# The first layers of two MLPs by Strassen's method with seven products, on tiles of 768 tokens, with streamed weights

## What is computed

```python
def _moe_ref(x, w1, w2, w3, w_out):        # 512 -> 1024 (twice), product, 1024 -> 1024 -> 512
    a = x @ w1
    b = x @ w2
    h = a * b @ w3
    return (h @ w_out).astype(np.float32)

def _moe2_ref(x, w_in, w_out):             # 512 -> 2048 -> 512
    h = x @ w_in
    g = h * (1.0 / (1.0 + np.exp(-h)))
    return (g @ w_out).astype(np.float32)
```

## Time and profile before

| | us |
|---|---|
| Median of 3 runs (lowest, highest) | 880.03 (879.86, 880.94) |
| The profiled execution's own time | 880.67 |
| Its span, first to last instruction | 878.9 |
| TensorE busy in the span | 858.4 |
| Attention phase | 0 to about 173 |
| First MLP, second MLP | 173 to about 474, about 474 to 876 |
| Mean granted clock of TensorE | 0.995 |

### The profile page before, as it was taken

The page is one execution under the profiler, slowest core; times in us unless marked ns, Lnnn a source line. Parts: engine busy times, 40 slices in busy tenths (PEclk is TensorE's granted clock), DMA queues, the critical chain, the costliest instruction groups (busy, mean ns, idle before and its releaser), DMA issues.

```text
span 878.9 us, 15422 instructions
## 1 busy us (share of the span) xinstructions
PE 858.4 (98%) x5872; PEld 792.3 (90%) x5872; DVE 317.5 (36%) x628; ACT 246.1 (28%) x584; POOL 143.8 (16%) x186
## 2 busy tenths in 40 slices
PE   5899999999999999999999999999999999999998
PEld 4678888899999999999999999999999999999997
DVE  4667777755212222121124432322222222322321
ACT  3656556433312222131224322111111111111211
POOL 5776566344000000000024000000000000000000
PEclk9899999999999999999999999999999999999999
DMA  7856665470000000000143000000000001000000
GB/s 192 207 128 160 172 160 141 100 204 0 2 1 0 0 0 0 0 1 1 49 139 100 1 1 37 1 1 36 0 0 36 0 0 37 1 0 33 4 1 37
DMA packets 90310, 43.54 MB, mean 50 GB/s; under 512 B 61856, under 2 KB 82848, under 8 KB 90272
## 3 DMA queue, kind: packets, MB, share of 16 engines
q1 hardware_dynamic: 90272, 43.01, 18.5%
HBM read 38.27 MB, written 4.72 MB: 49 GB/s over the span
## 4 chain that ended last, share of the span: by engine, by line
PE 94%; DVE 2%; POOL 1%; issue 1%; ACT 0%; DMA 0%; DVEq 0%; SPq 0%; POOLq 0%
PE ps L799 80%; PE ps L907 5%; PE ps L889 2%; PE ps L824 2%; PE ps L873 1%; PE ps L834 1%; PE ps L845 1%; PE ps L915 1%; POOL r L360 1%; PE ps L864 1%; PE ps L856 1%; DVE r L663 0%; DVE x L654 0%; DMA qn<-in_q 0%; DVE tot L701 0%
## 5 line engine op out<-in xcount | busy, mean ns | idle before, releaser
L799 PE MATMUL ps<-xs,r 128*128 128x384 f32 x2304 | 425.0, 335 | 0.1
L799 PEld LDWEIGHTS ps<-xs,r 128*128 128x128 f32 x2304 | 405.1, 188 | 8.7 <-issue 0.4
L799 PE MATMUL ps<-r,gh 128*128 128x512 f32 x576 | 194.9, 392 | 0.0
L585 ACT ACTIVATE gf<-ps 128x384 f32<-128x384 f32 x96 | 47.2, 492 | 320.0 <-PE ps L799 320.0
L766 DVE CAST gh<-gf 128x384 fp32r<-128x384 f32 x96 | 35.0, 364 | 281.6 <-ACT gf L585 274.7
L799 PEld LDWEIGHTS ps<-r,gh 128*128 128x128 f32 x576 | 108.1, 188 | 20.3 <-issue 0.2
L799 PE MATMUL ps<-r,gl 128*128 128x512 f32 x288 | 113.7, 395 | 0.0
L799 PE MATMUL ps<-gh,r 128*128 128x384 f32 x384 | 97.3, 334 | 0.0
L732 DVE TENSOR_TENSOR gf<-ps,osb 128x384 f32<-128x384 f32 x48 | 26.7, 557 | 186.7 <-ACT osb L431 186.7
L431 ACT ACTIVATE osb<-ps 128x384 f32<-128x384 f32 (+1 forms) x60 | 30.8, 513 | 194.9 <-PE ps L799 194.9
L799 PEld LDWEIGHTS ps<-gh,r 128*128 128x128 f32 x384 | 69.3, 188 | 0.0
(11 more groups left out here) (71 smaller groups left out, 648.4 us busy)
## 6 DMA issues: line engine op xcount, KB each, us to landing
raw<-in_moe_w_out SPq DMA_DIRECT2D x24, 256.0 KB, 3.0
qn<-in_q SPq DMA_DIRECT2D x32, 144.0 KB, 2.8
kn<-in_k SPq DMA_DIRECT2D x32, 144.0 KB, 3.2
vw<-in_v SPq DMA_DIRECT2D x32, 144.0 KB, 3.0
out<-osb SPq DMA_DIRECT2D x18, 256.0 KB, 2.0
wn<-in_moe_w SPq DMA_DIRECT2D x16, 256.0 KB, 3.2
raw<-in_moe_w SPq DMA_DIRECT2D x16, 256.0 KB, 4.5
raw<-in_moe_w_in SPq DMA_DIRECT2D x16, 256.0 KB, 4.9
```

What stands on the lines that cost most here:

```text
L585: nc.scalar.activation(gf[:, n % 2, :], ps[:, n % 2, 0:T], ACT.Silu).then_inc(g_ready, 1)
L799: e = nc.tensor.matmul(o, weights[a][l], tile[a][r], start=(first and a == 0 and p == 0), stop=(last and a == kk - 1 and p == 2))
```

## The change

T becomes 768, so there are three tiles. The first layers are computed by Strassen's method in Winograd's form. Tokens are cut in halves of 384, inputs in halves of 256 and output features in two blocks of 128; a **set** is such a 2 x 2 block product of seven products instead of eight. Each product is six matmuls of 384 columns. There are 24 sets in the first MLP (even k from w1, odd k from w2; 8 to a tile) and 24 in the second (8 to a tile).

- Weights are no longer kept: rw holds the raw blocks of a set (two buffers), loaded by SyncE, GpSimd makes four sums (`sums`), ScalarE the high parts of all seven factors (`weights_high`, 1792 columns in one operation) and GpSimd the low parts (`weights_low`, 1792 columns). The weights of the output layer are streamed in the same way (`out_weights_high`, `out_weights_low`).
- Tokens: seven factors a tile (xb). VectorE makes four sums (`sum_tokens`, `more_sums`), ScalarE all high parts (`tokens_high`), VectorE the low parts 0, 1, 3, 5 and GpSimd 2, 4, 6 (`tokens_low`), 768 columns each, during the last set of the tile before.
- The seven products use two PSUM banks in turn. ScalarE takes the first product (`take_m1`) and the first quarter (`take_c11`), VectorE adds the others up (`add`). TensorE waits before each product for what frees its bank.
- For the product a*b VectorE has `multiply` and `hidden_low` in odd sets, ScalarE `hidden_high`. In the second MLP it is `silu` and `split_g`.
- `L2_PARTS`, `L2_LAST` and `L4_PARTS` say how many parts of the following layer stand behind each product. A part of `l2` is three matmuls of 512 or of 256 columns, a part of `l4` three of 512.
- In the attention phase GpSimd has `sums(0)` at the head of the last step that computes scores, and the last step is put in another order on TensorE, ScalarE and VectorE. Buffers are laid out anew. The MLPs are written out without loops.

The diff, cut to what matters; 12 columns of indent are taken off:

```diff
-    T = 384
+    T = 768
+    TH = T // 2
+    PRODUCTS = 7
+    A_SLOT = (1, 4, 2, 5, 3, 0, 6)
+    QUARTERS = (0, 3, 2, 1)
+    GROUPS = TILES * MT // 2
+    SETS1 = 2 * GROUPS
+    SETS2 = TILES * FT // 2
+    SETS = SETS1 + SETS2
+    PER = 8
+    STAGES = SETS // PER
+    assert KT == HP == 4 and N % T == 0 and MT == PER and FT // 2 == PER
+    WIDE = 512
+    REST = T - WIDE
...
+        L2_PARTS = (0, 1, 2, 1, 2, 1, 2, 1, 2, 1, 2, 1, 0, 0)
+        L2_LAST = (0, 2, 3, 3, 3, 3, 2)
+        L4_PARTS = (1, 2, 2, 2, 2, 2, 1)
...
+def load_weights(k):
+    w = ((w1, w2)[k % 2] if k < SETS1 else w_in).rearrange("(k p) n -> p k n", p=P)
+    m, far = (k % PER // 2, MT // 2) if k < SETS1 else (k % PER, FT // 2)
+    after(sp, wa_lo, k - 1)
+    for b, n in ((0, m + far), (1, m)):
+        sp.dma_start(rw[:, k % 2, 2 * b:2 * b + 2, :].rearrange("p a (k c) -> p (a k) c", c=P),
+                     w[:, :, n * P:(n + 1) * P]).then_inc(rw_in[k % 2], 16)
...
+def sums(k):
+    blocks = rw[:, k % 2, :, :]
+    pool.wait_ge(rw_in[k % 2], 32 * (k // 2) + 32)
+    nc.gpsimd.tensor_tensor(blocks[:, 4, :], blocks[:, 0, :], blocks[:, 1, :], ALU.add
+                            ).then_inc(s1_ready, 1)
+    nc.gpsimd.tensor_tensor(blocks[:, 6, :], blocks[:, 2, :], blocks[:, 0, :], ALU.subtract
+                            ).then_inc(s3_ready, 1)
+    pool.wait_ge(s1_ready, k + 1)
+    nc.gpsimd.tensor_tensor(blocks[:, 5, :], blocks[:, 4, :], blocks[:, 2, :], ALU.subtract
+                            ).then_inc(s2_ready, 1)
+    pool.wait_ge(s2_ready, k + 1)
+    nc.gpsimd.tensor_tensor(blocks[:, 7, :], blocks[:, 3, :], blocks[:, 5, :], ALU.subtract
+                            ).then_inc(s4_ready, 1)
+def weights_low(k):
+    pool.wait_ge(wa_hi, k + 1)
+    nc.gpsimd.tensor_tensor(wa[:, k % 2, 1, :, :], rw[:, k % 2, 1:8, :],
+                            wa[:, k % 2, 0, :, :].bitcast(F32), ALU.subtract).then_inc(wa_lo, 1)
+def tokens_low(v, n):
+    pool.wait_ge(xb_hi, 7 * v + n + 1)
+    nc.gpsimd.tensor_tensor(xb[:, n, 1, :, :], tokens(v, n), xb[:, n, 0, :, :].bitcast(F32),
+                            ALU.subtract).then_inc(xb_lo[n], 1)
...
+    if not turn:
+        sums(0)
...
+tokens_low(0, 2)
+weights_low(0)
+tokens_low(0, 4)
+tokens_low(0, 6)
+for k in range(SETS):
+    if k + 1 < SETS:
+        sums(k + 1)
+        weights_low(k + 1)
+    if k >= SETS1:
+        out_weights_low(k - SETS1)
+    if k % PER == PER - 1 and k + 1 < SETS:
+        for n in (2, 4, 6):
+            tokens_low((k + 1) // PER, n)
...
+    if last:
         w3_high((MT - 1, 1), pT)
+        tokens_high(0, 1)
+        act.wait_ge(vt_ready, PAIRS)
+        tokens_high(0, 2)
+        act.wait_ge(scored, 2 * PAIRS)
+        act.wait_ge(pooled, 2 * PAIRS)
+        tokens_high(0, 3)
+        act.wait_ge(masked, PAIRS)
+        act.wait_ge(w3_turned, 2 * MT)
+        act.wait_ge(vd_ready, PAIRS)
+        weights_high(0)
...
+for k in range(SETS):
+    v, c, n = k // PER + 1, k % PER, k // 2
+    new = c == PER - 1 and v < STAGES
+    take_m1(k)
+    if k + 1 < SETS:
+        if k == 0:
+            act.wait_ge(w3_mul, MT)
+        weights_high(k + 1)
+    if new:
+        tokens_high(v, 0)
+    to_b = k < SETS1 and k % 2 == 1
+    if to_b:
+        hidden_high(n, 0)
+    else:
+        take_c11(k)
+    if new:
+        act.wait_ge(prod, PRODUCTS * k + 3)
+        tokens_high(v, 1)
+        tokens_high(v, 2)
+    if k >= SETS1:
+        out_weights_high(k - SETS1)
+        silu(k, 1)
+    elif to_b:
+        hidden_high(n, 1)
+    if new:
+        act.wait_ge(prod, PRODUCTS * k + 5)
+        tokens_high(v, 3)
+        tokens_high(v, 4)
+    if k < SETS1 and c == 1 and k > PER:
+        store_x2(k // PER - 1)
+    if k >= SETS1:
+        silu(k, 2)
+    elif to_b:
+        hidden_high(n, 2)
+    if new:
+        act.wait_ge(prod, PRODUCTS * k + 6)
+        tokens_high(v, 5)
+    if k >= SETS1:
+        silu(k, 3)
+    elif to_b:
+        hidden_high(n, 3)
+    if new:
+        act.wait_ge(prod, PRODUCTS * k + 7)
+        tokens_high(v, 6)
+    if k > SETS1 and c == 0:
+        store_out((k - SETS1) // PER - 1)
+    if k == SETS1:
+        store_x2(TILES - 1)
...
-        split_lo(0, 0, 0)
-        for m in range(HEAD // 2, HEAD):
-            r1_low(m)
+        more_sums(0)
+        tokens_low(0, 0)
+        tokens_low(0, 1)
+        tokens_low(0, 3)
         take_down()
...
+def add(k, i, o, term):
+    dve.wait_ge(prod, PRODUCTS * k + i + 1)
+    nc.vector.tensor_tensor(o, half_bank(k, i), term, ALU.add).then_inc(sum_ready, 1)
+def multiply(n, a):
+    q = QUARTERS[a]
+    dve.wait_ge(sum_ready, 5 * (2 * n + 1) + a + 2)
+    nc.vector.tensor_tensor(a4[:, q, :], mu[:, (0, 1, 0, 2)[q], :], a4[:, q, :], ALU.mult
+                            ).then_inc(h_mul, 1)
+def hidden_low(n, a):
+    q = QUARTERS[a]
+    to = slice(q % 2 * TH, (q % 2 + 1) * TH)
+    dve.wait_ge(h_hi, 4 * n + a + 1)
+    nc.vector.tensor_tensor(g[:, 1, n % 2, q // 2, to], a4[:, q, :], g[:, 0, n % 2, q // 2, to].bitcast(F32),
+                            ALU.subtract).then_inc(h_lo, 1)
...
+for k in range(SETS):
+    v, c, n = k // PER + 1, k % PER, k // 2
+    new = c == PER - 1 and v < STAGES
+    to_b = k < SETS1 and k % 2 == 1
+    dve.wait_ge(m1_ready, k + 1)
+    add(k, 1, mid, m1)
+    if to_b:
+        dve.wait_ge(prod, PRODUCTS * k + 3)
+        dve.wait_ge(c11_taken, n + 1)
+        nc.vector.tensor_tensor(a4[:, 0, :], half_bank(k, 2), a4[:, 0, :], ALU.mult
+                                ).then_inc(h_mul, 1)
+        dve.wait_ge(h_mul, 4 * n + 1)
+    add(k, 3, late, m1)
+    if new:
+        tokens_low(v, 0)
+    dve.wait_ge(sum_ready, 5 * k + 2)
+    add(k, 4, late if to_b else a4[:, 3, :], late)
+    if to_b:
+        multiply(n, 1)
+        hidden_low(n, 0)
+    elif k >= SETS1:
+        split_g(k, 0)
+    if new:
+        tokens_low(v, 1)
+    add(k, 5, m1 if to_b else a4[:, 2, :], m1)
+    if to_b:
+        multiply(n, 2)
+        hidden_low(n, 1)
+    elif k >= SETS1:
+        split_g(k, 1)
+    if new:
+        tokens_low(v, 3)
+    dve.wait_ge(sum_ready, 5 * k + 1)
+    add(k, 6, mid if to_b else a4[:, 1, :], mid)
+    if to_b:
+        multiply(n, 3)
+        hidden_low(n, 2)
+        hidden_low(n, 3)
+    elif k >= SETS1:
+        split_g(k, 2)
+        split_g(k, 3)
+    if new:
+        tokens_low(v, 5)
+    if c == 4 and v < STAGES:
+        sum_tokens(v)
+        more_sums(v)
+    if k < SETS1 and c == 1 and k > PER:
+        store_x2(k // PER - 1)
+    if k == SETS1:
+        store_x2(TILES - 1)
+    if k > SETS1 and c == 0:
+        store_out((k - SETS1) // PER - 1)
...
+def product(k, i):
+    v, c = k // PER, k % PER
+    if i == 0:
+        pe.wait_ge(wa_lo, k + 1)
+        after(pe, sum_ready, 5 * (k - 1) + 4)
+    elif i == 1:
+        after(pe, sum_ready, 5 * k)
+    elif i == 2:
+        pe.wait_ge(m1_ready, k + 1)
+    elif i == 4:
+        if k < SETS1 and k % 2 == 1:
+            pe.wait_ge(h_mul, 4 * (k // 2) + 1)
+        else:
+            pe.wait_ge(c11_taken, k - GROUPS + 1 if k >= SETS1 else k // 2 + 1)
+    else:
+        pe.wait_ge(sum_ready, 5 * k + {3: 1, 5: 2, 6: 3}[i])
+    if c == 0:
+        pe.wait_ge(xb_lo[i], v + 1)
+    for a in range(2):
         for p, (l, r) in enumerate(((0, 0), (1, 0), (0, 1))):
-            e = nc.tensor.matmul(o, weights[a][l], tile[a][r], start=(first and a == 0 and p == 0),
-                                 stop=(last and a == kk - 1 and p == 2))
-    return e
-def ab_part(i, n, z, a):
-    u, m = n // MT, n % MT
-    if z == 0 and a == 0:
-        if u == 0:
-            pe.wait_ge(r1_lo, 2 * m + 2)
-        pe.wait_ge(ab_ready, 2 * MT * i + n + 1)
-    e = product(ps[:, 2 * (n % 2) + z, 0:T], [[r1[:, 2 * m + z, l, a * P:(a + 1) * P] for l in range(2)]],
-                [[xs[:, u % 2, r, a, :] for r in range(2)]], a == 0, a == KT - 1,
-                (2 * i + u, a) if m == 0 and z == 0 else None)
-    if z == 1 and a == KT - 1:
-        e.then_inc(ab_done, 1)
+            e = nc.tensor.matmul(ps[:, (k + i) % 2, 0:TH], wa[:, k % 2, l, A_SLOT[i], a * P:(a + 1) * P],
+                                 xb[:, i, r, a, :], start=(i in (0, 1, 4) and a == 0 and p == 0),
+                                 stop=(a == 1 and p == 2), skip_group_check=True)
+    e.then_inc(prod, 1)
...
+        for a in range(4):
+            multiply(a)
+        multiply(0, (MT - 1, 1))
+        multiply(1, (MT - 1, 1))
         turn_local()
-        multiply(0)
-        multiply(1)
         turn_down()
-        multiply(2)
         weighted_local_waits()
-        multiply(3)
+        multiply(2, (MT - 1, 1))
+        multiply(3, (MT - 1, 1))
         weighted_local()
-        for a in range(4):
-            multiply(a, (MT - 1, 1))
         weighted_down()
-        for z in range(2):
-            for a in range(KT):
-                ab_part(0, 0, z, a)
         return
...
+for k in range(SETS):
+    for i in range(PRODUCTS):
```

(12 more changed lines are left out.)

566 lines of the change are left out of this document (265 added, 301 removed).

## The result

| | before | after |
|---|---|---|
| Median, us | 879.94 | 923.38 |
| Lowest to highest, us | 878.31 to 880.94 | 922.19 to 927.55 |
| Profiled execution's own time (span), us | 880.67 (878.9) | 927.55 (925.7) |

Before's median is here that of its runs beside after's. The ratio is 1.0499, 95% interval 1.0464 to 1.0533. The forecast was 892, with a range of 866 to 909: the sign was right, the size wrong. The profiled execution is the slowest of after, 4 us above its median; against before's it is 46.9 us longer, where the sum said 11.7.

A forecast was written before the change was run, and what follows sets the result against it. TensorE, busy 98% of the span, was taken to bound the kernel. -49.9 + 12 + 16 + 6 + 1.6 + 4 + 5 + 17 = +11.7 us on 880.67 gave 892.4, forecast 892, range 866 to 909.

The forecast's parts named there:

- Matmuls times interval, -49.9: First layers of both MLPs: 288 fewer matmuls of 384 columns at 0.1733 us each save 49.9 us.
- rival b: Second layer of the first MLP: narrow 256-column matmuls cost 0.158 us each, adding 12 us, to 904; chance 0.08.
- Holds on VectorE: VectorE operations with two SBUF inputs wait for GpSimd operations to end; adds, which read PSUM, do not.
- ordinary pair: Two sets of the first MLP without a tile change: 1.5 us lost in each of eight, +12 us.
- Changes of the first MLP: Tile changes at sets 7 to 8 and 15 to 16: product 4 starts late, 8 us each, +16 us.
- Start: Attention's end and first sets: first product at 179.2 us, set 1 at 193.9, +17 us (10 to 22).
- Second MLP, ordinary sets: 0: Second MLP: each add is done 1 us or more ahead because 12 output parts lie between products; 0 us.
- +5 for both: Second MLP, sets 31 and 39: tokens_low come between, walked at 0 to 3.5 us; 5 us for both.
- Clock, 0 in the sum: TensorE's clock falling after waits was left out of the sum and kept only as a rival, chance 0.12.
- (a): Queues keep up: VectorE's two-SBUF-input operations wait little for GpSimd, all lower ends hold, 867 us; chance 0.25.
- (c): Waits at tile changes and start lower TensorE's clock three to five times, +6 to +15 us, up to 907; chance 0.12.
- (d): Whole kernel: the sums cancel the saving within 1.8 us; chance 0.05.

The follow-up runs named there:

- a2_spread: The changed kernel with VectorE's four token sums in the second MLP put one each behind sets 2 to 5 of a tile: 909.92 us, ratio 1.0336 to before.
- a1_sums_first: The changed kernel with GpSimd computing the sums for the set after next ahead of the last tokens_low at four tile changes: 908.14 us, ratio 1.0311 to before.
- c1_wait_long: The kernel before with TensorE made to wait six times in the second MLP for a GpSimd addition of 1024 columns: 908.42 us, ratio 1.0302.
- a14_x2: Reordered changed kernel (spread sums, new start, serving new sets first), with next-layer parts dealt later where they wait for x2 copies: 876.55 us, ratio 0.9948 to before.
- a6_all: The changed kernel with four order edits together (GpSimd sums first, token sums spread, start reordered, l2 parts dealt out evenly): 890.34 us, ratio 1.0108 to before.
- a11_adds: The kernel with four order edits, plus VectorE's add of product 6 ahead of hidden_low(1) and tokens_low(3) at every tile change: 908.54 us, ratio 1.0303 to before.

## Why the prediction was wrong in size

- **Matmuls times interval, -49.9**: right. The 256-wide ones cost what their columns say (rival b, 0.158 each, fell): in the timeline of after three of them start at 300.56 and the next work at 300.91, 0.117 each.
- **Holds on VectorE**: right as a mechanism, adds free and operations with two SBUF inputs held. No row of before showed one behind 4 us; L739 took 4.81 us in place of 0.95 behind one of 4.28. That agrees with the Trainium skill (SBUF — State Buffer, "SBUF: two separate sides"), by which the other "fully blocks". The ordinary pair was 30% too dear: at the end of set 3 only the first hidden_low and the first multiply were held, where I had them held behind every sum.
- **Changes of the first MLP**: 13.3 for 16, but not by the one wait that was walked. Of the 6.7 us of a change, 2.5 stand ahead of product 4 behind a4, where I had all of it, 6.0 to 9.6; the rest is VectorE's adds ahead of products 0 and 1. The sign that I had named, gaps of 3 us or more behind a4, didn't come; that the sum of a change came out near is partly luck.
- **Start**: 14.1 for 17. The first product was walked rightly (178.56 against 179.2). That set 1 starts at 194.07, as forecast (193.9), is luck: I had it wait for weights_low(1), which ended at 193.00 with TensorE still at work. What delayed it were the waits of products 3 and 4 of set 0 and 2.3 us of slow clock, which the sum hadn't. Up to there gaps cost 10.8 where I had 13.2, and the end of set 1 cost 3.3 where I had 5.5.
- **"Second MLP, ordinary sets: 0"**: this step failed. The 12 parts of the output layer do cover the adds, but the set in which the token sums stand isn't ordinary: 10.5 us. a2_spread shows it.
- **"+5 for both" changes of the second MLP**: mis-sized, 11.2. The walk stopped at VectorE and left out the late sums (a1_sums_first brings the two to 5.3) and the copies to osb.
- **Clock, 0 in the sum**: this step failed most, 20.0 us. I treated the fall as a rival of 3 to 5 times with a price of 2 to 3 us; it was twelve times at 1.55 to 2.3. Eight of the twelve lie at places that my own sum had as waits: the start, sets 8, 16 and 24, and the copies of x2 in sets 10, 18 and 25. Two more are at sets 29 and 37, two at the changes of the second MLP. With 1.55 on each of the twelve, the sum would have been near 30 instead of 12. The Trainium skill (TensorE: Matmul & The Clock Gate, "Why this matters for your kernels") warns of idle gaps between bursts; I weighed it, and gave it 0.12. The gaps of 2.5 to 2.7 us that brought the clock down in c1_wait_long are shorter than those it warns of, and the measurement decides. c1_wait_long also shows the price.
- **What offset what**: clock +20.0, sets 29 and 37 +10.5, changes of the second MLP +6.2 and smaller gaps +8 over the forecast; ordinary pairs -3.6, start -2.9, changes of the first MLP -2.7 under it. The waits alone, without the clock, sum to 69 us against the 49.9 saved, so the sign doesn't hang on the clock.
- **Rivals**: (a) the queues keep up: fell. That the queues can be made to keep up well enough is shown by a14_x2, with edits of order only. (c) was right as a mechanism, with 20.0 us where it had 6 to 15, and ran on top of the forecast, not in its place. (d), the sums cancelling, fell with the sign. I had put the forecast's losses and the clock's as alternatives, though the one causes the other.

## What to carry to other kernels

A gap ahead of TensorE of 2.5 us or more costs itself and, mostly, 1.6 us of slow clock: put both into the sum for each one, and count the gaps just under 2 us as open (four of 1.7 to 1.9 us in after were followed by a fall, two of 1.8 us weren't). When work leaves the bounding engine and goes to the others, walk every distinct set of the program, including the one that prepares the next tile, and look for operations of two SBUF inputs on VectorE that can meet a long GpSimd operation. Such losses are mostly losses of order: here some 47 us went by moving instructions, none by saving any, and 42 us of gaps are left.

## What the runs showed that I had not expected

The same gap doesn't always bring the clock down: 2.55 us ahead of 598.48 did, 2.55 ahead of 741.28 didn't, gaps of 1.8 and 1.9 us in sets 10 and 18 did in after and not in a6_all, and the 2.3 us ahead of product 4 of sets 8 and 16 didn't in after. What decides it stays open.

An edit that serves one wait can cost far more than it gives: a11_adds moved three gaps of 3.2 us by one product, made two of 7.2, and its kernel was 17 us slower. Each wait has to be followed to what is late next, in every place where the edit applies.
